# Chunk 1's diagonal blocks in a buffer of their own, scaled by GpSimd; two weight halves, the scores and the keys of chunk 2 in other places on VectorE

## What is computed

```python
def _attn_ref(q, k, v, beta):
    k_n = k / (np.linalg.norm(k, axis=-1, keepdims=True) + 1e-06)
    state = np.zeros((B, H, D, D), dtype=np.float32)
    for t in range(S):
        kt, vt, bt = (k_n[:, :, t], v[:, :, t], beta[:, :, t, None])
        y[:, :, t] = np.einsum('bhd,bhde->bhe', q[:, :, t], state)
        v_old = np.einsum('bhde,bhd->bhe', state, kt)
        state = state + bt[:, :, :, None] * np.einsum('bhd,bhe->bhde', kt, vt - v_old)

x = y.transpose(0, 2, 1, 3).reshape(B * S, H * D)
h = x @ w_in;   g = np.maximum(h, 0.0) + np.log1p(np.exp(-np.abs(h)));   x = g @ w_out
h = x @ w_in2;  out = (h * np.cos(h)) @ w_out2
```

## Time and profile before

| | us |
|---|---|
| median of 3 runs | 1040.71 |
| lowest and highest | 1040.28, 1044.33 |
| the profiled execution | 1041.15 |
| its span, first to last instruction | 1038.30 |
| TensorE busy | 992.5 (96%) |
| VectorE busy | 720.9 (69%) |
| ScalarE busy | 508.8 (49%) |
| GpSimd busy | 332.6 (32%) |

### The profile page before, as it was taken

The page is one execution under the profiler, slowest core; times in us unless marked ns, Lnnn a source line. Parts: engine busy times, 40 slices in busy tenths (PEclk is TensorE's granted clock), DMA queues, the critical chain, the costliest instruction groups (busy, mean ns, idle before and its releaser), DMA issues.

```text
span 1038.3 us, 26229 instructions
## 1 busy us (share of the span) xinstructions
PE 992.5 (96%) x11480; PEld 849.1 (82%) x11480; DVE 720.9 (69%) x1092; ACT 508.8 (49%) x819; POOL 332.6 (32%) x406
## 2 busy tenths in 40 slices
PE   4878799999999999999999999999999999999998
PEld 3776678788878788887788888999999999999997
DVE  4968567768586858655644676777768777687775
ACT  3554463563455355435544545545445445454443
POOL 2079548902960592088000586100101001010000
PEclk9569899999999999999999999999999999999999
DMA  9212113101210210011003421002010020010101
GB/s 213 53 50 78 32 48 63 47 2 34 48 47 18 47 48 17 18 34 47 8 11 91 162 83 61 1 2 61 1 39 23 1 61 1 2 29 1 31 1 30
DMA packets 100768, 42.66 MB, mean 41 GB/s; under 512 B 76560, under 2 KB 96016, under 8 KB 100656
## 3 DMA queue, kind: packets, MB, share of 16 engines
q1 hardware_dynamic: 96064, 39.73, 15.1%
q10 hardware_dynamic: 4592, 1.28, 0.6%
HBM read 31.56 MB, written 9.44 MB: 39 GB/s over the span
## 4 chain that ended last, share of the span: by engine, by line
PE 86%; DVE 5%; POOL 4%; issue 2%; ACT 2%; DMA 0%; SPq 0%; DVEq 0%; POOLq 0%
PE wide L1564 9%; PE wide L1565 8%; PE wide L1566 8%; PE wide L1588 4%; PE wide L1589 4%; PE wide L1590 4%; PE bank L1565 4%; PE bank L1566 4%; PE bank L1564 4%; PE wide L1584 3%; PE wide L1586 3%; PE wide L1585 3%; PE bank L1586 3%; PE bank L1585 3%; PE bank L1584 3%; PE bank L1588 2%
## 5 line engine op out<-in xcount | busy, mean ns | idle before, releaser
L1564 PE MATMUL wide<-x_hi,wi_hi 128*128 128x512 f32 x408 | 166.2, 407 | 0.5 <-DVE x_lo L943 0.5
L1566 PE MATMUL wide<-x_hi,wi_lo 128*128 128x512 f32 x408 | 160.2, 393 | 0.0
L1565 PE MATMUL wide<-x_lo,wi_hi 128*128 128x512 f32 x408 | 160.1, 392 | 0.0
L1150 DVE TENSOR_TENSOR g_lo<-tmp,g_hi 128x512 fp32r<-128x512 f32 x192 | 154.3, 804 | 6.6
L805 ACT ACTIVATE tmp<-wide 128x512 f32<-128x512 f32 x88 | 52.6, 598 | 204.8 <-PE wide L1566 204.8
L1141 DVE SCALAR_TENSOR_TENSOR tmp<-wide,tmp 128x512 f32<-128x512 f32 x88 | 60.6, 689 | 129.4 <-ACT tmp L809 129.1
L505 POOL TENSOR_TENSOR inv<-inv,blk 128x31 f32<-128x31 f32 (+15 forms) x155 | 116.5, 751 | 12.1
L1148 DVE CAST g_hi<-tmp 128x512 fp32r<-128x512 f32 x192 | 98.1, 511 | 20.2 <-DVE tmp L1144 0.5
L525 POOL TENSOR_TENSOR x_lo<-x_raw,x_hi 128x1536 fp32r<-128x1536 f32 x6 | 23.0, 3834 | 269.2 <-ACT x_hi L562 269.2
L1131 DVE TENSOR_SCALAR tmp<-tmp 128x512 f32<-128x512 f32 x96 | 53.7, 559 | 70.2 <-ACT tmp L796 70.2
L502 POOL TENSOR_TENSOR blk<-blk,inv 128x31 f32<-128x31 f32 (+15 forms) x155 | 96.4, 622 | 13.6 <-DVE blk L1042 1.2
(11 more groups left out here) (184 smaller groups left out, 2205.8 us busy)
## 6 DMA issues: line engine op xcount, KB each, us to landing
stage<-in_moe_w_in SPq DMA_DIRECT2D x32, 192.0 KB, 3.3
stage<-in_moe_w_out SPq DMA_DIRECT2D x8, 768.0 KB, 4.6
qn<-in_q SPq DMA_DIRECT2D x24, 192.0 KB, 3.7
x_t<-x_res SPq DMA_DIRECT2D x6, 768.0 KB, 3.6
x_raw<-x_t SPq DMA_DIRECT2D x6, 768.0 KB, 5.7
res_v<-in_v SPq DMA_DIRECT2D x22, 192.0 KB, 3.7
out_x<-res SPq DMA_DIRECT2D x20, 192.0 KB, 3.0
kn<-in_k SPq DMA_DIRECT2D x32, 96.0 KB, 3.0
```

The source lines that it names most:

```text
L1150: nc.vector.tensor_tensor(lo, g, hi.bitcast(FP32), ALU.subtract).then_inc(g_ready, 1)
L1564: mm(dst, wi_hi[:, ft, kt, :], hi[:, kt, :], start=(kt == 0), stop=False)
L1565: mm(dst, wi_hi[:, ft, kt, :], lo[:, kt, :], start=False, stop=False)
L1566: last = mm(dst, wi_lo[:, ft, kt, :], hi[:, kt, :], start=False, stop=(kt == KT - 1))
```

## The change

- Chunk 1's diagonal blocks get a tile of their own, `blk_1`, in memory that later holds high weights of piece 6; ScalarE therefore waits for the end of `substitute(1)` before it writes these.
- With that, `take_diagonal(1)` stands right behind `turn_inverse(0)` on VectorE, in front of the copies of the inner products.
- The scaling of these blocks moves from VectorE to GpSimd (`scale_blocks(1)`), and GpSimd's two low halves (pieces 0 and 1) move to VectorE, behind the last delta of chunk 0 and in front of `x_lo`.
- ScalarE's high half of piece 3 moves from the end of `first()` to the start of `attention(1)`, behind two `main`s.
- `take_p(1, "P0")` stands in front of `factors(2)`, and the scaled keys of chunk 2 are cut off from it (`scale_keys`) and stand one `main` later.

```diff
--- before.py
+++ after.py
@@ -125,6 +125,8 @@
     with ExitStack() as early:
         sb("soon_in", [P, FT * DM // 2], where=early)
         m1_0 = sb("m1_0", [P, 2, U, BLK], where=early)
+        sb("soon_in_next", [P, BLK * BLK], where=early)
+        blk_1 = sb("blk_1", [P, BLK, BLK], where=early)
     wi_hi = sb("wi_hi", [P, FT, KT, P], F32R)
     with ExitStack() as early:
         sb("soon_in_lo", [P, FT * DM // 2], where=early)
@@ -244,6 +246,10 @@
 
 
         return need if c == 0 else 8 + 4 * (c - 1) + need
+
+    def blocks_of(c):
+
+        return blk_1 if c == 1 else blk
 
     def values_of(c, s):
 
@@ -488,12 +494,13 @@
             nc.gpsimd.memset(flat(inv[:, :, :])[:, 0:BLK * BLK:BLK + 1], 1.0).then_inc(inv_clean, 1)
 
         def scale_blocks(c):
+            blk = blocks_of(c)
             pool.wait_ge(blk_set, blocks_until(c))
             nc.gpsimd.tensor_tensor(blk[:, :, :], blk[:, :, :],
                                     beta_blk[:, :].unsqueeze(1).to_broadcast([P, BLK, BLK]), ALU.mult).then_inc(sub_step, 1)
 
         def substitute(c):
-            n = 62 * (c - 1) + 1
+            n, blk = 62 * (c - 1) + 1, blocks_of(c)
             pool.wait_ge(inv_clean, 2 * c + 2)
             for j in range(BLK - 1):
                 prod = blk[:, 0:j + 1, j + 1:BLK].rearrange("p c i -> p i c")
@@ -525,15 +532,9 @@
             nc.gpsimd.tensor_tensor(flat(x_lo[t % 2][:, :, :]), x_raw[t % 2][:, :],
                                     flat(x_hi[t % 2][:, :, :]).bitcast(FP32), ALU.subtract).then_inc(x_lo_set, 1)
 
-        def first_low_weights(n):
-            hi, lo = halves(pieces1, n)
-            pool.wait_ge(w_hi_set, n + 1)
-            nc.gpsimd.tensor_tensor(lo, staged(STAGE1, stage1, pieces1, n), hi.bitcast(FP32), ALU.subtract).then_inc(w_split, 1)
-
         clean(0)
         clean(1)
-        for n in range(2):
-            first_low_weights(n)
+        scale_blocks(1)
         substitute(1)
         pool.wait_ge(w_split, EARLY)
         for n in range(EARLY, NP):
@@ -720,11 +721,12 @@
             take_x(0, 0, "YT0")
             take_late_x()
             take_upper(1, 1, "S1")
-            high_weights(3)
 
         def attention(c):
             after = c + 1 < NCH
-            if 1 < c < NCH - 1:
+            if c == 1:
+                high_weights(3)
+            elif c < NCH - 1:
                 root(c + 1)
             yield
             take_transposes(c, "Q0", qT)
@@ -758,6 +760,7 @@
             yield
             yield
             if c == 1:
+                act.wait_ge(inv_ready, 2)
                 high_weights(6)
             yield
             yield
@@ -890,7 +893,7 @@
 
             turn_beta(c)
             dve.wait_ge(blocks_filled, 4 * c + 4)
-            nc.vector.transpose(blk[:, :, :].rearrange("p i (x o) -> p i x o", o=2),
+            nc.vector.transpose(blocks_of(c)[:, :, :].rearrange("p i (x o) -> p i x o", o=2),
                                 wide[c][:, :].rearrange("p (o x i) -> p i x o", o=2, i=BLK)).then_inc(blk_set, 1)
 
         def take_blocks(c, g):
@@ -957,7 +960,11 @@
             nc.vector.tensor_scalar(norm[:, 2, :], norm[:, 2, :], 0.5, 1e-6, ALU.mult, ALU.add).then_inc(norm_step, 1)
             step(5)
             nc.vector.reciprocal(norm[:, 2, :], norm[:, 2, :]).then_inc(norm_step, 1)
-            step(6)
+            if c != 2:
+                scale_keys(c)
+
+        def scale_keys(c):
+            dve.wait_ge(norm_step, c * 6 + 6)
             g = 2 * c % 4
             for s in ((0,), (1,)) if c == 0 else ((0, 1),):
                 keys = kn[:, g + s[0]:g + s[-1] + 1, :, 0:D]
@@ -1035,18 +1042,17 @@
         def first():
             take_inverse(0)
             turn_inverse(0)
+            take_diagonal(1)
             take_inner(0, 0)
             take_inner(0, 1)
-            take_diagonal(1)
-            dve.wait_ge(blk_set, blocks_until(1))
-            nc.vector.tensor_tensor(blk[:, :, :], blk[:, :, :],
-                                    beta_blk[:, :].unsqueeze(1).to_broadcast([P, BLK, BLK]), ALU.mult).then_inc(sub_step, 1)
             dve.wait_ge(consts_set, 3)
             take_delta(0, 0, "V0")
             mask_scores("P0", pT)
             take_rest(0, 1, "KS1")
             mask_scores("P1", late_pT)
             take_delta(0, 1, "V1")
+            low_weights(0)
+            low_weights(1)
             take_x(0, 0, "YT0")
             take_late_x()
             low_weights(2)
@@ -1065,11 +1071,15 @@
                 low_weights(3)
             yield
             if c == 1:
+                take_p(1, "P0")
+            yield
+            if c == 1:
                 factors(2)
-            yield
-            take_p(c, "P0")
-            yield
-            if c == 1:
+            else:
+                take_p(c, "P0")
+            yield
+            if c == 1:
+                scale_keys(2)
                 take_rest(1, 0, "KS0")
             yield
             take_inverse(c)
```

2 lines of the change are left out of this document (1 added, 1 removed).

## The result

| | before | after |
|---|---|---|
| median, us | 1040.53 (17 runs) | 1038.22 (17 runs) |
| lowest and highest | 1039.59, 1044.33 | 1036.90, 1041.43 |
| ratio, 95% interval | | 0.9975 (0.9967 to 0.9983) |
| the profiled execution | 1041.15 | 1038.22 |

What follows compares the result with a forecast made beforehand. GpSimd's substitution for chunk 1 was taken as the bound: starting 5.14 us earlier less 2.9 lost to low halves gives 2.2. 1041.15 less 2.2 is 1038.9, less 0.44 is 1038.4 to 1038.5; range 1035.0 to 1041.4.

Steps and rivals of the forecast that it cites:

- The bound: GpSimd's substitution for chunk 1, from 64.12 to about 113.6, sets the stage's time through VectorE; TensorE starts 5.94 us after it.
- The start, 5.14 us earlier: GpSimd's substitution for chunk 1 starts at 58.98 in place of 64.12, with transposes ending at 56.31 and scaling of 2.37 us.
- The loss to two low halves, 2.9 us: GpSimd's solve loses 1.44 us to each low half on VectorE, 2.9 in all, with bounds of nothing and 3.5.
- The sum, 2.2: 5.14 less 2.9: solve and the product behind it come 2.2 us earlier, and all later work moves by the same amount.
- x_lo up to 0.9 late: The low halves on VectorE may put x_lo and the first product1 up to 0.9 us later, covered by TensorE's idle time.
- Scores moved, not won: TensorE's 3.00 us stall before the state product mostly moves before the keys' transposes; 1.6 us stay won but count as nothing.
- TensorE idle 5.5 us, then half clock: Before the product behind chunk 1's inverse TensorE idles 5.5 us in place of 6.08, then half clock follows as before.
- Weights of piece 3: SyncE issues the load at 73.4, ScalarE makes the high half at 83 to 84; nothing counted.
- the clock staying up: Rival, chance 0.18: 5.5 us idle doesn't bring TensorE's clock down, 4.1 us at 0.50 become about 2.05; time 1036.4.
- GpSimd loses nothing: Rival, chance 0.13: the two low halves on VectorE cost GpSimd nothing; gain 5.14 us, time 1035.6, with the clock up 1033.5.
- The solve ends as before: Rival, chance 0.09: GpSimd's solve starts earlier but loses 5.1 us and ends as before; time 1040.7.
- TensorE the bound: Rival, chance 0.06: low clock from near 102 makes TensorE reach the product at 120.4, past 119.6; slower, 1042.4 up to 1047.

Runs made afterwards that it cites:

- e3: Changed kernel with the low halves of weight pieces 0 and 1 taken away but for 16 of 1536 columns; ratio to the kernel before 0.9939.
- e5: Changed kernel with the scaling of chunk 1's blocks back on VectorE, right behind the transposes; ratio to the kernel before 0.9948.
- e8: Changed kernel with the two low halves back on GpSimd in front of its scaling, which stays there; ratio to the kernel before 1.0020.
- e2: Changed kernel with the scores of chunk 1 behind the norms and keys again, all else kept; ratio to the kernel before 0.9975.
- e6: Changed kernel with TensorE's product1(5) of tile 0 done four times, to fill its wait; ratio to the kernel before 0.9964.
- e1: Kernel before with only the scores of chunk 1 moved before the norms and chunk 2's keys one main later; ratio to it 1.0003.
- e4: Changed kernel with each of the two low halves made twice on VectorE; ratio to the kernel before 0.9985.
- e7: Changed kernel with the scaling on VectorE behind the transposes and product1(5) done three times; ratio to the kernel before 0.9950.
- e11: Changed kernel with product1(5) done three times, 18 matmuls more; ratio to the kernel before 0.9948.
- e9: Changed kernel with VectorE's take_inverse(1) moved behind main(4) and the masked scores of chunk 2; ratio to the kernel before 0.9948.

## Why the prediction was right, point by point

- **The bound**: right. In the changed kernel, too, GpSimd's last step releases VectorE and this TensorE, which starts 5.96 us behind it (5.98 before, or 5.94 counted from VectorE's start, as the prediction did). e3, e5 and e8 move the start or the length of the solve, and the time goes the same way each time. In the traces the end of the solve and the inner products move together in e3 (3.0 and 3.2 us earlier) and e5 (2.0 and 2.0); in e8 they are 0.75 and 0.2 us later than before.
- **The start, 5.14 us earlier**: 5.55 measured. The transposes ended at +3.05 where 3.45 was worked out (1.1 us behind the turned inverse, not the 1.53 they took behind the copies); the scaling took 2.34 (2.37 predicted).
- **The loss to two low halves, 2.9 us**: the solve grew by 3.48 us in this profile, by 2.5 to 3.7 over all kernels that share the halves, and e3 takes 3.04 of it back. The one row (1.44) was a better guide than the bound of 3.5; in the trace the two steps lost 1.6 and 1.4 us, 3.0 in all. Another 0.4 us are a term that the prediction put at nothing: the two masks of the scores, which it said cost GpSimd what they did, now meet other steps of the solve and cost it 2.1 us in place of 1.7 (by the lengths of the steps beside them, against the shortest of the same step in all traces). The rule of the Trainium skill, page "SBUF — State Buffer", section "Who interferes with whom", would give 1.75 each: it agrees in kind, and e3 gives 1.52 each.
- **The sum, 2.2**: 2.07 at the end of the solve, 2.09 at the product, 1.9 in the span, 2.6 by the ratio. The start was 0.4 under, the loss 0.6 under in this profile; they nearly cancelled, so the sum is better than its terms, by luck. Behind the product the prediction let everything move by the same amount; in the traces the lead grew from 2.09 to 2.8 us at `main(8)`. That is the clock, which the prediction expected to be the same: from the product to the inner products it took 3.83 us in place of 4.11, and the inner products 2.21 in place of 2.66 (a granted 0.58 over the 4.1 us, before 0.50).
- **x_lo up to 0.9 late**: wrong in sign. The first product came at +23.77, before +24.73. TensorE waited 1.19 us for it but had got there sooner. The deltas of chunk 0 ended 0.8 us earlier (+18.0, before +18.8), where the prediction counted nothing for the scaling that is gone. With the halves away (e3) the first product came at +23.0, so the delay by the halves, 0.8, is there. It can't be read finer than 1 us: in kernels with the changed kernel's order up to there it came at +23.6 to +24.6 (e2, e6), and at +25.1 in e5, where VectorE does the scaling.
- **Scores moved, not won**: right, with 3.14 us of new wait (1.4 or more predicted); e1 and e2 show it from both sides.
- **TensorE idle 5.5 us, then half clock**: 6.53 us, and half clock (0.58 on average from 117.3 to 121.4). It arrived at +58.1 instead of +59.0.
- **Weights of piece 3**: issued at 72.34 (73.4 predicted), high half at 82.58 (83 to 84), no wait.
- **The rivals**: the clock staying up got 0.18 and did not happen in the changed kernel, but it is real: e4, e6, e7 and e11 show it, 1.6 us at the nine matmuls, 1.8 at `main(8)` and 2.8 by the ratio of e11, against the 2.05 of the prediction. "GpSimd loses nothing" is refuted by e3, "The solve ends as before" by its end 2.07 us earlier, "TensorE the bound" by 6.53 us of idle.

What stays open: how much of the gain of e5 is the clock (its only profile is of its slowest execution), what the 2.1 us of e8 are, and what decides whether a short wait brings the clock down. 1.44 us did in e9 and 1.68 us did not in e4. The wait of 3.14 us in front of the keys' transposes even went both ways: the granted clock from 100 to 106 is 1.00 in the changed kernel and 0.72 in e9 and e11, with the same wait in front of the same work.
